# Second turns of k and q moved beside step 3's turns of P, in the same PSUM banks

## What is computed

```python
def _attn_ref(q, k, v):                  # each (4, 8, 576, 64): 4 sequences, 8 heads
    scores = scale * np.matmul(q, k.transpose(0, 1, 3, 2))
    mask = block_i >= block_j            # blocks of 64 positions: 9 of them
    scores = np.where(mask, scores, -1000000000.0)
    scores = scores - np.max(scores, axis=-1, keepdims=True)
    attn = np.exp(scores)
    attn = attn / (np.sum(attn, axis=-1, keepdims=True) + 1e-09)
    return np.matmul(attn, v)

x = attention, heads side by side: (2304, 512)
x = _moe_ref(x)      # h = x @ w_in (512 x 2048); (h - tanh(h)) @ w_out
x = _moe2_ref(x)     # out = x; where x @ w_skip > 0:
                     #   out += gate * relu(x @ w1[e]) @ w2[e], e = argmax(x @ w_gate)
```

## Time and profile before

| | |
|---|---|
| median of 3 runs | 799.75 us (798.41 to 800.69) |
| the profiled execution, whole | 798.25 us |
| its span, first to last instruction | 796.7 us |
| TensorE busy | 778.5 us, 98% |
| weight loads busy | 606.1 us, 76% |
| VectorE, ScalarE, GpSimd busy | 502.2, 297.4, 251.3 us |
| mean granted clock of TensorE | 0.998 |

### The profile page before, as it was taken

One profiled execution on the slowest core, in us unless ns is written; L12 is line 12 of the kernel. 1 busy time (PEld: TensorE's weight loads), 2 busy tenths in 40 slices (PEclk: granted clock), 3 DMA queues, 4 the chain that ended last, 5 costly groups with the idle time before them and its releaser, 6 DMA issues.

```text
span 796.7 us, 14950 instructions
## 1 busy us (share of the span) xinstructions
PE 778.5 (98%) x4600; PEld 606.1 (76%) x4601; DVE 502.2 (63%) x1242; ACT 297.4 (37%) x738; POOL 251.3 (32%) x307
## 2 busy tenths in 40 slices
PE   6999999999999999999999999999999999999996
PEld 3555556555888888888888888888997888888885
DVE  4887888776543276665766566754557565656653
ACT  3676777676101121113011221112226254655642
POOL 4767676766870000002000100002221233333333
PEclk9999999999999999999999999999999999999999
DMA  8333444321337250001000010000172375565564
GB/s 169 87 94 92 107 117 101 90 73 42 103 83 2 2 172 0 1 1 53 0 0 0 0 54 1 0 1 1 54 196 82 112 242 203 197 220 183 186 213 145
DMA packets 88154, 69.27 MB, mean 87 GB/s; under 512 B 66962, under 2 KB 66962, under 8 KB 88104
## 3 DMA queue, kind: packets, MB, share of 16 engines
q1 hardware_dynamic: 83160, 62.93, 29.7%
q0 software_dynamic: 3760, 5.38, 2.0%
q10 hardware_dynamic: 1184, 0.30, 0.2%
HBM read 62.97 MB, written 8.84 MB: 90 GB/s over the span
## 4 chain that ended last, share of the span: by engine, by line
PE 69%; DMA 16%; issue 6%; DVE 3%; POOL 3%; POOLq 2%; ACT 0%; SPq 0%; DVEq 0%
PE psum L1361 46%; DMA xg<-out_dram,rec_next 7%; PE psum L1309 7%; PE psum L1331 7%; PE psum L1280 6%; DMA out_dram<-y_rows,rec_now 4%; PE psum L1265 3%; DMA out_dram<-y_rows,rec_early 2%; POOL rec_next L626 1%; DMA xg_third<-out_dram,rec_early 1%; DMA lists<-rec,slot_i 1%; POOLq L392 1%; PE psum L1453 1%; DVE neg_max L897 1%; DMA q_rows<-in_q_dram 1%
## 5 line engine op out<-in xcount | busy, mean ns | idle before, releaser
L795 ACT ACTIVATE g<-psum 128x512 f32<-128x512 f32 (+1 forms) x80 | 44.4, 555 | 306.9 <-PE psum L1361 306.9
L1099 DVE TENSOR_TENSOR g<-psum,g 128x512 f32<-128x512 f32 (+1 forms) x80 | 51.0, 637 | 157.3 <-ACT g L795 157.1
L580 POOL DMA_INDIRECT lists<-rec,slot_i x18 | 18.7, 1038 | 331.5 <-DVE slot_i L1033 327.5
L555 POOL TENSOR_SCALAR probs<-probs,row_inv 128x384 f32<-128x384 f32 (+2 forms) x96 | 99.0, 1040 | 59.6 <-DVE row_inv L904 59.6
L1361 PE MATMUL psum<-x_hi,wi_hi 128*128 128x512 f32 x256 | 100.1, 391 | 0.0
L1361 PE MATMUL psum<-x_hi,wi_lo 128*128 128x512 f32 x256 | 99.7, 389 | 0.0
L1361 PE MATMUL psum<-x_lo,wi_hi 128*128 128x512 f32 (+1 forms) x256 | 99.6, 389 | 0.0
L698 ACT ACTIVATE probs<-psum,neg_max 128x576 f32<-128x576 f32 (+2 forms) x144 | 74.5, 526 | 20.5 <-DVE neg_max L897 17.5
L1129 DVE TENSOR_TENSOR we<-w_half,we x96 | 59.5, 690 | 33.5 <-ACT we L681 33.5
L1361 PE MATMUL psum<-wo_hi,g_hi 128*128 128x512 f32 x192 | 74.9, 390 | 0.1
L1361 PE MATMUL psum<-wo_lo,g_hi 128*128 128x512 f32 x192 | 74.7, 389 | 0.0
(11 more groups left out here) (229 smaller groups left out, 1488.0 us busy)
## 6 DMA issues: line engine op xcount, KB each, us to landing
w_half<-in_moe_w_dram SPq DMA_DIRECT2D x64, 512.0 KB, 4.3
q_rows<-in_q_dram SPq DMA_DIRECT2D x32, 144.0 KB, 3.0
out_dram<-x_rows SPq DMA_DIRECT2D x18, 256.0 KB, 2.1
k_rows<-in_k_dram SPq DMA_DIRECT2D x30, 144.0 KB, 3.3
v_rows<-in_v_dram SPq DMA_DIRECT2D x32, 128.0 KB, 2.3
w_raw<-in_moe_w_in_dram SPq DMA_DIRECT2D x16, 256.0 KB, 3.6
w_raw<-in_moe_w_out_dram SPq DMA_DIRECT2D x16, 256.0 KB, 2.6
wide_x<-w_rows SPq DMA_DIRECT2D x4, 256.0 KB, 5.3
```

What stands on the lines that cost most here:

```text
L555: pool.tensor_scalar(p, p, row_inv[:, j, m:m + 1], None, ALU.mult).then_inc(short_normed, 1)
L1099: dve.tensor_tensor(g_f, h_at(f, first, last), g_f, ALU.subtract).then_inc(g_done, 1)
```

## The change

The second part of k's and q's turns goes to columns 256 to 447 of its bank (`TURN_AT`), behind the 256 columns of step 3's turns of P. In pairs 1 to 14, TensorE does the two P turns of `a_ps`, the two k turns, the two P turns of `d_ps` and the two q turns in one group in front of step 2's scores. The k and q turns no longer wait for the copies of step 3's P. As a bank may not be read while it is written, the copies of step 3's P now wait until the k or q turns of the same bank are done. VectorE's copy of q moves from behind step 2's maxima to in front of them. Pair 0, which has no P turns before it, keeps its order, and the last pair has no next one.

```diff
+    TURN_AT = [0, 2 * P]
+    assert TURN_AT[1] + SEQ - TURNED[1] <= 512
...
             def keys_out(u, n):
                 act.wait_ge(act_full, A_TURN["k", u, n])
-                high(kt[:, u % 2, TURNED[n]:TURNED[n + 1]], a_ps[:, 0:TURNED[n + 1] - TURNED[n]]).then_inc(act_free, 1)
+                high(kt[:, u % 2, TURNED[n]:TURNED[n + 1]],
+                     a_ps[:, TURN_AT[n]:TURN_AT[n] + TURNED[n + 1] - TURNED[n]]).then_inc(act_free, 1)
...
             def first_out(u, j):
-                act.wait_ge(act_full, A_TURN["p", u, j])
+                act.wait_ge(act_full, A_TURN["k", u + 2, 1] if j == 3 and u + 2 < PAIRS else A_TURN["p", u, j])
...
             def second_out(u, j):
-                dve.wait_ge(dve_full, D_TURN["p", u, j])
+                dve.wait_ge(dve_full, D_TURN["q", u + 2, 1] if j == 3 and u + 2 < PAIRS else D_TURN["p", u, j])
...
                 if u > 0:
                     second_out(u - 1, 3)
+                    if more:
+                        queries_out(u + 1, 1)
                 most(u, 2)
-                if more:
+                if more and u == 0:
                     queries_out(u + 1, 1)
...
             def turn_rows_of(rows, u, n, bank):
...
                 for m in range((TURNED[n + 1] - TURNED[n]) // QT):
-                    last = pe.transpose(bank[:, QT * m:QT * m + QT], rows[:, u % 2, TURNED[n] // QT + m, :], ident[0:QT, 0:QT])
+                    at = TURN_AT[n] + QT * m
+                    last = pe.transpose(bank[:, at:at + QT], rows[:, u % 2, TURNED[n] // QT + m, :], ident[0:QT, 0:QT])
...
             def turn_keys(u, n):
-                act_bank(A_TURN["k", u, n])
+                if not (n == 1 and u >= 2):
+                    act_bank(A_TURN["k", u, n])
...
             def turn_queries(u, n):
-                dve_bank(D_TURN["q", u, n])
+                if not (n == 1 and u >= 2):
+                    dve_bank(D_TURN["q", u, n])
...
                     turn_first(u - 1, 3)
+                    if more:
+                        turn_keys(u + 1, 1)
                     turn_second(u - 1, 3)
+                    if more:
+                        turn_queries(u + 1, 1)
                 score(u, 2)
-                if more:
+                if more and u == 0:
                     turn_keys(u + 1, 1)
                     turn_queries(u + 1, 1)
```

More of the change, by code:

```diff
@@ L882, in queries_out @@
                 dve.wait_ge(dve_full, D_TURN["q", u, n])
-                dve.tensor_scalar(qt[:, u % 2, TURNED[n]:TURNED[n + 1]], d_ps[:, 0:TURNED[n + 1] - TURNED[n]],
+                dve.tensor_scalar(qt[:, u % 2, TURNED[n]:TURNED[n + 1]], d_ps[:, TURN_AT[n]:TURN_AT[n] + TURNED[n + 1] - TURNED[n]],
                                   SCALE, None, ALU.mult).then_inc(dve_free, 1)
```

## The result

| | before | after |
|---|---|---|
| median of 5 runs | 799.01 us (797.73 to 800.69) | 793.63 us (793.23 to 794.88) |
| profiled execution, its span | 796.7 us | 791.9 us |
| ratio | | 0.9943, 95% interval 0.993 to 0.9956 |

What follows compares the result with a forecast made beforehand. TensorE's own back-to-back stream was taken to bound attention's 14 changed pairs. Saving 0.148 us of border a pair, other terms zero, gave 799.75 - 2.07 = 797.7 us, 0.26% less; range 796.3 to 800.2.

Steps and rivals of the forecast that it cites:

- The border price: In 14 changed pairs, one way into the turns and one out of them go: 0.148 us a pair, 2.1 us less.
- The borders of 96 rows: Inside the new group, three changes a pair between 128-row and 96-row turns: taken as nothing, upper bound 0.15 us each.
- The first rival: Inside the new group, 96-row turns are a form of their own: 0.30 us a pair slower, 804.0 us; chance 0.06.
- The waits in the pair: In a changed pair, scores start 0.33 us sooner or later without stalling TensorE: VectorE has 0.29 spare, ScalarE 0.52.
- the second rival: In a changed pair, the later scores make TensorE wait: 0.18 us more a pair, 2.5 us, 802.3 us; chance 0.05.
- The two waits that go (step 3): Before k's and q's second turns, TensorE's waits for ScalarE's and VectorE's copies of P go: priced at zero.
- What comes after moves as a whole (step 8): After attention, everything starts 2.1 us earlier as a whole; no transfer with its own time was known to end last.
- The median started from: Whole kernel: before's median taken as 799.75 us, 1.5 above the profiled execution; the forecast subtracts 2.07 from it.

## Why the prediction was right or wrong

**The border price: right.** It was worked out as 0.148 us a pair from groups of two sizes and measured as 0.143. The Trainium skill (TensorEngine Tiling (Array Packing), Key Properties) has a change of tiling mode drain the engine; the runs agree, with 0.143 us gained for one change of form less, and with nothing gained when only k's half moved, where the turns moved and the number of borders stayed.

**The borders of 96 rows: right**, taken as nothing, measured as 0.003 to 0.004 us. The first rival (804.0) had this as its condition and falls.

**The waits in the pair: right.** The room forecast for VectorE (0.29) and ScalarE (0.52) was found as 0.36 and 0.51, and the second rival (802.3) with its wait is in no trace.

**The two waits that go (step 3): wrong as to what they are.** I priced them as time at their place, nothing, and for their place that is right. They are also 28 instructions of the program, and with them a fetch of TensorE's instructions moves by 6.8 us against the transfers around it, nearly 400 us after the last pair. The prediction doesn't look at the fetches at all, though the page's list of queues has them, and doesn't ask where after attention a wait on a transfer stands.

**What comes after moves as a whole (step 8): this is the step that failed.** I wrote that no transfer with a time of its own ends last. One does: TensorE waits 1.98 us for the early gather in the profiled execution, and the page of before has `DMA xg_third<-out_dram,rec_early` in the chain of work that ended last, though TensorE is busy for 98% of the span. Its price in the first two traces is 2.2 us, more than the pairs. Of that, some 1 us belongs to the program (0.93 in the traces, 1.1 in the medians of all runs: 3.1 less 2.0), with the spread told above, and the rest to the one execution. The term should have been: pairs 2.0, and 0 to 2 us more for a wait that stands in before and may go or stay.

**The median started from.** 799.75 was a median of three runs; 136 runs have 797.97. From there the forecast would have been 795.9, and the changed kernel's 794.86 is 1.0 under it. The 0.57% of the first set is in part luck of the set: all runs together give 3.1 us, 0.39%. The range was built on the scatter of three runs and on rivals in attention alone; the wait at the experts' start was visible and would have widened it downward.

**Open:** by what way the fetch's place lengthens the `rec_early` loads, if it is this fetch that does it. It holds back a packet of the weight loads 8 us ahead; what that does to the small loads wasn't followed. Since other fetches move with it, no run moves this one alone. The kernel with only k's half moved, with the fetch late, one wait of 4.27 and a median near before's, says that it is not the only cause.

## What to carry to other kernels

Where one engine is back to back, price a change of its order by borders: take two groups of the same instructions in different number, and what doesn't scale is the border. Then go through the rest of the trace for waits on transfers behind the edited stretch, above all short ones of a microsecond or two: an edit that only shifts or shortens the program can move these by as much as it gains. A gain under half a per cent needs the kernel before run again on the same chip, dozens of times, and a control that changes the length of the program without its work.

## What was not expected of the hardware

- Leaving out 28 waits that were already met made a kernel of 798 us faster by 2.4 and, in a second set, by 1.3 us (ratios 0.9976 and 0.9981), with no period changed in the stretch where they stood. With only k's half moved, 14 instructions fewer and the fetch at the same late place, the median over 25 runs was only 0.6 us lower.
- A 16 KB fetch of instructions took 0.93 to 0.95 us about 6 us into the weight loads, 2 us ahead of the last `rec_early` load, and 2.5 to 2.9 us where it began 0.2 to 0.4 us ahead of them.
- After waits of 2.27, 2.36 and 2.92 us the granted clock was 0.50 for the stretch behind them; after one of 1.98 us it stayed at 1.00.
- Eight matmuls took 1.97 or 1.08 us at the kernel's start, as the clock rose at 18.0 or 14.3 us; over all traces of both families it rose between 12.0 and 18.9 us.
